# First gated pair reordered: next sums ahead of w_out's low parts, a low part of g behind a sum, one tile less to wait for, stores in two groups

## What is computed

```python
# 1. attention with 4 sink keys and a window of 128, q, k, v of (2, 8, 768, 64)
x = attention(q, k, v)                       # 1536 tokens x 512
# 2. mixture of experts: every token goes to one of 8 experts, 192 tokens each
h = np.maximum(x[mask] @ w1[e], 0.0)         # 512 -> 1024
x[mask] = h @ w2[e]                          # 1024 -> 512
# 3. gated product
a = x @ w_a                                  # 1536 x 1536
b = x @ w_b
return (a * b @ w_out).astype(np.float32)    # 1536 x 512
```

## Time and profile before

| | |
|---|---|
| median of 3 runs | 627.31 us (627.05 to 628.0) |
| the profiled execution, its own time | 627.19 us |
| its span in the trace | 625.5 us |
| PE busy | 582.8 us (93%) |
| DVE, ACT, POOL busy | 416.9, 316.0, 338.0 us |
| mean granted TensorE clock | 0.965 |

### The profile page before, as it was taken

One profiled execution on the slowest core, in us unless ns is written; L12 is line 12 of the kernel. 1 busy time (PEld: TensorE's weight loads), 2 busy tenths in 40 slices (PEclk: granted clock), 3 DMA queues, 4 the chain that ended last, 5 costly groups with the idle time before them and its releaser, 6 DMA issues.

```text
span 625.5 us, 11118 instructions
## 1 busy us (share of the span) xinstructions
PE 582.8 (93%) x3818; PEld 525.6 (84%) x3820; DVE 416.9 (67%) x1079; ACT 316.0 (51%) x766; POOL 338.0 (54%) x408
## 2 busy tenths in 40 slices
PE   8999999994359999999999899999999999999995
PEld 4888778863239999999999899999999999999984
DVE  3889669847845777678994567747746656656663
ACT  3788669742304776677875444534524334424410
POOL 6211101100012602269877999997997798687613
PEclk9999999996559999999999999999999999999999
DMA  9995060505012865676762132222222422220002
GB/s 186 269 208 127 14 182 27 161 27 161 1 53 69 280 224 191 226 236 208 249 218 73 54 96 73 82 68 69 69 68 67 168 63 73 67 67 3 34 1 101
DMA packets 87674, 72.12 MB, mean 115 GB/s; under 512 B 40000, under 2 KB 74816, under 8 KB 87616
## 3 DMA queue, kind: packets, MB, share of 16 engines
q1 hardware_dynamic: 83888, 64.64, 35.1%
q0 software_dynamic: 1920, 6.29, 2.9%
q10 hardware_dynamic: 1808, 0.44, 0.4%
HBM read 65.08 MB, written 6.29 MB: 114 GB/s over the span
## 4 chain that ended last, share of the span: by engine, by line
PE 77%; DVE 10%; POOL 7%; ACT 3%; issue 2%; ACTq 1%; DVEq 0%; POOLq 0%
PE psum L1883 11%; PE psum L1962 8%; PE psum L1965 8%; PE psum L1964 8%; PE psum L1876 5%; PE psum L1878 5%; PE psum L1877 5%; PE psum L1685 5%; PE psum L1884 5%; PE psum L1647 4%; POOL w_lo L779 3%; PE psum L1668 3%; PE psum L1624 2%; DVE above L1340 2%; DVE w_lo L1103 1%
## 5 line engine op out<-in xcount | busy, mean ns | idle before, releaser
L779 POOL TENSOR_TENSOR w_lo<-w_raw,w_hi 128x512 fp32r<-128x512 f32 x96 | 110.2, 1181 | 25.2 <-ACT w_hi L996 25.1
L1883 PE MATMUL psum<-h_hl,w_hi 128*128 128x384 f32 x256 | 75.4, 363 | 0.9 <-POOL w_lo L702 0.6
L1883 PE MATMUL psum<-x_hl,w_hi 128*128 128x384 f32 x256 | 73.5, 359 | 0.3 <-DVE x_hl L1475 0.3
L1964 PE MATMUL psum<-x_hl,w_hi 128*128 128x384 f32 x216 | 72.3, 335 | 0.0
L863 ACT ACTIVATE w_hi<-w_raw 128x1024 fp32r<-128x1024 f32 (+1 forms) x72 | 69.1, 960 | 0.0
L1103 DVE TENSOR_TENSOR w_lo<-w_raw,w_hi 128x1024 fp32r<-128x1024 f32 x44 | 65.1, 1479 | 0.0
L1600 DVE TENSOR_TENSOR o_acc<-psum,o_acc 128x512 f32<-128x512 f32 x60 | 41.3, 690 | 35.2 <-PE psum L1878 35.2
L1884 PE MATMUL psum<-h_hl,w_lo 128*128 128x192 f32 x256 | 64.1, 250 | 0.0
L1884 PE MATMUL psum<-x_hl,w_lo 128*128 128x192 f32 x256 | 64.1, 250 | 0.0
L687 POOL CAST p_sink<-p_sb 128x16 fp32r<-128x16 f32 x40 | 8.2, 205 | 98.7 <-ACT p_sb L884 78.3
L1962 PE MATMUL psum<-t_first,w_hi 128*128 128x384 f32 x168 | 56.5, 336 | 2.0 <-DVE psum L1563 1.5
(11 more groups left out here) (236 smaller groups left out, 1530.1 us busy)
## 6 DMA issues: line engine op xcount, KB each, us to landing
w_raw<-in_moe_w_dram SPq DMA_DIRECT2D x32, 1024.0 KB, 5.5
w_raw<-in_moe_w_a_dram SPq DMA_DIRECT2D x12, 512.0 KB, 3.6
w_raw<-in_moe_w_b_dram SPq DMA_DIRECT2D x12, 512.0 KB, 3.5
w_raw<-in_moe_w_out_dram SPq DMA_DIRECT2D x12, 512.0 KB
k_raw<-in_k_dram SPq DMA_DIRECT2D x16, 192.0 KB, 4.4
v_sb<-in_v_dram SPq DMA_DIRECT2D x16, 192.0 KB, 4.2
xs_scratch<-x_rows SPq DMA_DIRECT2D x8, 384.0 KB, 3.4
q_raw<-in_q_dram SPq DMA_DIRECT2D x14, 192.0 KB, 4.4
```

The lines of the kernel that those rows point to most:

```text
L779: return nc.gpsimd.tensor_tensor(out_t, t, hi_t.bitcast(f32), ALU.subtract)
L1883: nc.tensor.matmul(bk[:, 0:2 * CAP], lhs_hi, rhs_both, start=first, stop=False)
L1964: nc.tensor.matmul(o, w_h, t_lo[:, t, :], start=False, stop=False, skip_group_check=True)
```

## The change

Four edits:

1. **POOL, stage 0.** `split_out(0)` stood between `split_mix(1, 0)` and `add_blocks(0, 1)`; it now stands behind `split_mix(0, 1)`, as in all later stages.
2. **DVE, stage 0.** `lower_b(0, 0)` stood ahead of the sum L1563; it now stands behind it.
3. **PE, `down(n)`.** The first tile waits for one kept tile less of the `down` before; the second tile waits for the last.
4. **POOL, stages 6 and 7.** `store_rows` takes a range of tiles. Tiles 0 to 2 of the first half are stored at the end of stage 6, tiles 3 to 5 in stage 7 between `add_blocks(1, 7)` and `split_mix(1, 7)`. The second half is stored as before.

```diff
-            def store_rows(ct):
-                for st in range(TILES_C):
+            def store_rows(ct, tiles):
+                for st in tiles:
                     pool.wait_ge(down_kept, TILES_C * (PAIRS_F * (ct + 1) - 1) + st + 1)
                     nc.gpsimd.indirect_dma_start(
...
                 add_blocks(1, n)
+                if n == PAIRS_F + 1:
+                    store_rows(0, range(TILES_C // 2, TILES_C))
                 split_mix(1, n)
-                if n == 0:
-                    split_out(0)
                 if n + 1 < STAGES:
                     add_blocks(0, n + 1)
                     split_mix(0, n + 1)
-                if n > 0:
-                    split_out(n)
+                split_out(n)
                 if n in T_ADDED:
                     split_t(1, T_ADDED.index(n))
                 if n == PAIRS_F:
-                    store_rows(0)
-            store_rows(1)
+                    store_rows(0, range(TILES_C // 2))
+            store_rows(1, range(TILES_C))
...
                 nc.vector.tensor_tensor(u3_sb, yb, p1_sb, ALU.add).then_inc(b_made, 1)
-                lower_b(n, 0)
+                if n > 0:
+                    lower_b(n, 0)
                 dve.wait_ge(products_b, 7 * n + P5)
                 dve.wait_ge(b_made, 9 * n + 3)
                 nc.vector.tensor_tensor(w, zb, u3_sb, ALU.add).then_inc(b_made, 1)
+                if n == 0:
+                    lower_b(n, 0)
...
                     if st == 0 and n > 0:
-                        pe.wait_ge(down_kept, TILES_C * n)
+                        pe.wait_ge(down_kept, TILES_C * n - 1)
                     elif st == 1:
+                        if n > 0:
+                            pe.wait_ge(down_kept, TILES_C * n)
                         pe.wait_ge(a11_kept, mixed)
```

## The result

The changed kernel takes 622.88 us (median of 5, 621.52 to 623.54) against 627.09 us before (median of 5, 626.13 to 628.0): ratio 0.993, 95% interval 0.9913 to 0.9947. That is 4.2 us less, with 3.3 to 5.5 us inside the interval; 623.8 was forecast, with a range of 622.3 to 625.1. The profiled execution took 623.54 us, with a span of 621.8 us.

The account below looks back on a forecast made before the run. PE sets the pace of part 3, so time can only be won where it stands still. From 627.19 us, 2.31 (stage 0) and 1.11 (the end) were subtracted, giving 623.77, stated as 623.8, range 622.3 to 625.1.

Parts of the forecast that it names:

- Stage 0: 2.31 us: POOL going straight to the sums lets PE start mix(0, 1) sooner, removing both stage 0 waits: 2.31 us gained.
- Edit 2 costs nothing at best: Stage 0, DVE: edit 1 alone removes both stalls; lower_b(0, 0) behind the sum delays later sums by at most 0.56 us.
- POOL's lead shrinks without harm: After stage 0, POOL's lead over PE, taken at mix(0, 2), falls from 7.1 to 4.8 us; PE gives nothing back.
- DVE's and POOL's shared reads: Stage 0 low parts: POOL keeps pace beside DVE's PSUM-reading instructions, gain 2.31; if they contended too, 1.7 us.
- The end: 1.11 us: down(11) starts 1.04 us sooner by waiting for one kept tile less, and its 0.07 us restart goes: 1.11 us gained.
- Edit 4: 0 in the sum: Splitting the stores: effect on the L1539 stall in mix(0, 7) left at 0, bounds -1.07 and +1.07 us.
- the late count goes too: Rival: breaking up the six stores also removes the mix(0, 7) stall, 1.07 us, giving 622.7; chance 0.26.
- the likeliest case: Whole kernel: the forecast itself, 623.8 us, own range 623.3 to 624.3, chance 0.50.
- The slower rival: Stores land too late for keep_down(6), stopping PE in down(6); over 628.6 us needs landing at 512; slower or equal 0.04.
- the three cases below 626.06: Whole kernel: forecast 0.50, late count gone too 0.26, stage 0 gives less or a second late count 0.14.
- The rule that was weighed beside this rival: Stores: all engines' DMAs interleave on the same 16 DMA engines, so a pause would make 622.7 likelier.

Follow-up runs that it names:

- the run with the load held back: Edits 1 to 3, six stores in a run, SP issuing stage 7's w_out load later, against the kernel before: 624.08 us, ratio 0.9948.

## Why the prediction was right, and what it missed

**Stage 0: 2.31 us.** Right. Edit 1 alone gives 2.28 in its profile and 2.24 in time, the full change 2.38. PE was expected 0.1 us ahead of POOL at `mix(0, 1)` and is (0.07). The chain from POOL's detour over ACT's queue to DVE's sum is what the rows said: taking away only its last link (edit 2 alone) moves the wait and gains nothing.

**Edit 2 costs nothing at best.** Right: without it the kernel is the same within 0.1 us.

**POOL's lead shrinks without harm.** Right: no wait behind L779 in stages 1 to 4 in any run with edit 1. From `mix(0, 1)` to `mix(0, 7)` before and after take the same time within 0.01 us.

**DVE's and POOL's shared reads.** The low parts of `mix(0, 1)` take 4.50 us, while the DVE instructions beside them read one operand from PSUM; those beside L1589 took 5.09. The Trainium skill (SBUF — State Buffer, section Who interferes with whom) says that DVE's `tensor_tensor`, which these instructions are, contends with GpSimd's reads when both its inputs are in SBUF, and not when at most one is. This case's trace agrees, and the 0.6 us held open for it were not spent. No run here changes this one thing alone.

**The end: 1.11 us.** Right: 1.04 + 0.07 in the profile, 1.16 in time for the edit alone (0.3 to 1.8 by its interval).

**Edit 4: 0 in the sum.** This step fell, and it is the term that was mis-sized: "From these rows alone I can't tell, nor whether it is in each execution. I leave it at 0 in the sum". It is in each profile with six stores in a run: seven with a wait of PE (0.6 to 0.8 us), and the eighth, all six in stage 7, with the late count alone. It is in none of the five kernels with three and three, nor with four and two. It is worth 1.06 us in this pair of profiles (0.9 to 1.1 in all seven), and 1.66 in time alone (0.6 to 2.1). So the case that came true was the rival "the late count goes too", 622.7, which had a chance of 0.26; 622.88 was measured, below the 623.3 to 624.3 of the likeliest case. That the whole range holds it is owed to the rival. A hint was in the rows: both engines resumed together, right behind the last store, once in twelve stages. That made a cause likelier than chance, and the runs then showed it.

**The slower rival** had a bound of 5.7 us for the landing. The packets show 2.4 us before and 1.4 after, so it never came near.

**Two slips** changed nothing. The second tile of `down(11)` was due at 611.18 and kept at 610.71, which is 0.47 us to spare and not 0.3. And the three cases below 626.06 add up to a chance of 0.90 for faster, not 0.91.

What stays open: by which path a run of indirect DMAs holds back PE's counts. The load ahead isn't it, and the instruction packet isn't. The number in a run matters: six do it, four didn't in the one execution of it; five wasn't tried. The rule that was weighed beside this rival (the Trainium skill, DMA: Bandwidth & Descriptors, section Issuing engines are not separate DMA queues) pointed to the right time, but the run with the load held back speaks against interleaving with that load as the reason, and no run shows another use of those engines as the reason.

## What to carry to other kernels

- Two waits of one engine a few microseconds apart may be one delay. Follow both back to the first instruction that is late; removing the nearer cause alone can move the wait and gain nothing (0.0 us here, against 2.3 us for the farther one).
- When engines with nothing else in common resume at the same moment after a wait for an engine that never paused, look at what a third one, or the DMA queues, did just before. Here six indirect DMAs in a run did it; a pause after three (or after four, in the one execution of it), or another place for them, gives 1 us back.
- At a boundary between two groups of tiles, wait for the tile whose bank is needed and not for the group: one constant, 1.1 us.

## What the runs showed of the hardware

**Late counts.** With six indirect stores issued back to back (7.4 us), semaphore counts of PE's products come up to 2.2 us late, while PE's matmuls go on at 0.17 us. ACT and DVE resume together, 1.1 to 1.3 us after the last issue ends. The trace also keeps the time of each semaphore update, and it tells where the delay arises. In the kernel before, the last matmuls of P2, P7 and P5 of `mix(0, 7)` end at 497.42, 498.46 and 499.50 (modelled); their updates stand at 499.57, 499.64 and 499.72, all within 0.15 us. In the changed kernel each update that the trace has for these products stands within 0.02 us of that end. POOL's own update for its first sum, in the midst of the delay, is on time (499.10, 499.11). So ACT and DVE aren't slow to react: it is PE's updates that are held back, and then come in one burst. In all eight profiles the first product that is held back for long (1.8 to 2.2 us) is one whose last matmul ends just after the sixth issue begins, by 0.06 to 0.3 us; after the fifth, the one delay seen was 0.3 us.

**A stall may cost the clock too.** With edit 4 alone, PE has the same two waits in stage 0 as before, but its granted clock then falls to the lower level (0.5 of full speed, 1.2 GHz) for a while, and matmuls start 0.32 us apart in place of 0.17. The stretches of busy time of that kernel (length, PE, PEld, DVE, ACT, POOL, granted clock, DMA share, GB/s):

```profile
354.00:356.00 2.00, 1.43 (x7) 1.11 (x8) 1.93 (x5) 0.74 (x2) 1.86 (x3) 1.00 0.04 8
356.00:358.00 2.00, 2.00 (x8) 2.00 (x9) 1.67 (x4) 0.44 (x2) 2.00 (x3) 0.59 0.42 93
358.00:360.00 2.00, 2.00 (x9) 2.00 (x8) 0.27 (x1) 1.51 (x4) 1.24 (x3) 0.56 1.06 393
360.00:362.00 2.00, 2.00 (x13) 2.00 (x12) 0.84 (x3) 1.13 (x3) 1.58 (x2) 1.00 0.11 39
```

and of the kernel before, run once more, with the same waits:

```profile
356.00:358.00 2.00, 1.54 (x9) 1.21 (x8) 1.97 (x5) 0.98 (x2) 1.86 (x3) 1.00 0.04 8
358.00:360.00 2.00, 2.00 (x14) 2.00 (x13) 1.37 (x4) 1.22 (x3) 1.92 (x4) 1.00 0.67 214
```

`mix(0, 1)` then takes 8.95 us in place of 7.42 from its first matmul to `down(0)`: 1.5 us on top of what the waits cost. It happened in two of the five profiles that have the waits of stage 0 (edit 2 alone and edit 4 alone) and in none of the nine that don't. So few can't show that the waits are the cause. The timed executions point the same way: the profile of edit 2 alone has a mean granted clock of 0.959 and took 629.12 us, and three executions of the kernel before have 0.959 too and took 629.03 to 629.27 us, 2 us above its medians. Those four are among 91 executions of kernels with the waits; of the 47 of kernels without them, none has a mean below 0.961. But a mean doesn't tell in which part of the kernel the clock was low, and every profile has a stretch at the lower level long before part 3 (0.50 at 150 to 155 us, in both kernels). That the gain in timed executions holds some of this is likely, and not shown.
